# One landing buffer instead of two for the gathered token rows

## What is computed

```python
kv  = einsum('bhsd,bhse->bhde', k, v); out = einsum('bhsd,bhde->bhse', q, kv)
x   = (out / rms(out) * g_norm)  reshaped to (4608, 512)

logits = x @ w_gate + modality_bias[modality_id]        # 8 experts
e_idx  = argmax(logits);  gate_w = softmax(logits)[e_idx]
for e in range(8):                                      # each token goes to one expert
    h = maximum(x[e_idx == e] @ w1[e], 0)               # 512 -> 1024
    out[e_idx == e] = gate_w * (h @ w2[e])              # 1024 -> 512

out = (sigmoid(x @ w_gate2) * (x @ w_val)) @ w_out      # 512 -> 1536 -> 512
```

## Time and profile before

| | |
|---|---|
| median of 3 runs | 1508.95 us |
| the profiled execution's own time | 1508.95 us, of which its span 1507.2 us and 1.75 us around it |
| PE busy | 1386.6 us, 92% of the span |
| DVE busy | 906.8 us, 60% |
| ACT busy | 442.5 us, 29% |
| POOL busy | 303.1 us, 20% |
| granted clock, mean over the span | 0.956 |

### The profile page before, as it was taken

One profiled execution on the slowest core, in us unless ns is written; L12 is line 12 of the kernel. 1 busy time (PEld: TensorE's weight loads), 2 busy tenths in 40 slices (PEclk: granted clock), 3 DMA queues, 4 the chain that ended last, 5 costly groups with the idle time before them and its releaser, 6 DMA issues.

```text
span 1507.2 us, 25225 instructions
## 1 busy us (share of the span) xinstructions
PE 1386.6 (92%) x8270; PEld 1141.1 (76%) x8271; DVE 906.8 (60%) x1509; ACT 442.5 (29%) x766; POOL 303.1 (20%) x364
## 2 busy tenths in 40 slices
PE   4776379999999999979899999999999999999997
PEld 4565358878888888757678888888888888888885
DVE  3565776677758784456775557555575555655541
ACT  4555122222222222324432214211142112422221
POOL 0055324444444444212110001100011000110011
PEclk9777689999999999979999999999999999999999
DMA  9783256577747765459967443374426544144420
GB/s 329 290 311 126 88 163 183 169 211 212 204 147 223 208 197 146 121 128 354 336 233 202 147 151 121 128 201 147 147 78 168 173 158 155 42 175 147 147 77 28
DMA packets 132433, 262.68 MB, mean 174 GB/s; under 512 B 20200, under 2 KB 85736, under 8 KB 126208
## 3 DMA queue, kind: packets, MB, share of 16 engines
q1 hardware_dynamic: 71200, 199.41, 39.7%
q10 hardware_dynamic: 49952, 32.50, 8.3%
q0 software_dynamic: 11200, 29.69, 5.9%
HBM read 179.44 MB, written 51.73 MB: 153 GB/s over the span
## 4 chain that ended last, share of the span: by engine, by line
PE 80%; DVE 6%; DMA 5%; issue 4%; ACT 3%; SPq 1%; DVEq 1%; ACTq 0%; POOL 0%; POOLq 0%
PE ps L1547 30%; PE ps L1527 18%; PE ps L1497 13%; PE ps L1484 12%; DMA mixes<-mix 2%; PE ps L1406 2%; PE ps L1419 2%; PE ps L1517 1%; PE ps L1383 1%; DMA graw<-in_moe_w_val 1%; DMA vt<-in_v 1%; DMA raw<-in_moe_w 1%; DVE ew L957 1%; ACT qp L726 1%; DVE ew L963 0%
## 5 line engine op out<-in xcount | busy, mean ns | idle before, releaser
L1547 PE MATMUL ps<-a_hi,st 128*128 128x512 f32 x1344 | 421.5, 389 | 0.8 <-DVE u L1328 0.8
L1547 PEld LDWEIGHTS ps<-a_hi,st 128*128 128x128 f32 x1344 | 252.3, 188 | 54.0 <-DVE a_lo L1289 1.5
L1527 PE MATMUL ps<-wo,shi 128*128 128x512 f32 x864 | 268.5, 392 | 6.2 <-DVE slo L1298 5.4
L1547 PE MATMUL ps<-a_lo,st 128*128 128x512 f32 x672 | 261.4, 389 | 0.0
L1484 PE MATMUL ps<-ew,xhi 128*128 x640 | 200.3, 394 | 12.1 <-DVE xlo L1144 12.1
L1497 PE MATMUL ps<-ew,hhi 128*128 x640 | 200.8, 395 | 9.1 <-DVE hlo L1169 9.1
L1527 PEld LDWEIGHTS ps<-wo,shi 128*128 128x128 f32 x864 | 162.5, 189 | 44.4 <-issue 5.2
L671 POOL DMA_INDIRECT out<-ot,out_tok x36 | 35.9, 998 | 717.7 <-ACT ot L834 711.9
L1527 PE MATMUL ps<-wo,slo 128*128 128x512 f32 x432 | 170.0, 393 | 0.0
L1484 PEld LDWEIGHTS ps<-ew,xhi 128*128 128x128 f32 x640 | 122.0, 191 | 38.3 <-issue 12.9
L1497 PEld LDWEIGHTS ps<-ew,hhi 128*128 128x128 f32 x640 | 121.9, 191 | 35.9 <-issue 10.4
(11 more groups left out here) (221 smaller groups left out, 1811.8 us busy)
## 6 DMA issues: line engine op xcount, KB each, us to landing
st<-mixes SPq DMA_DIRECT2D x48, 1792.0 KB, 7.2
raw<-in_moe_w SPq DMA_DIRECT2D x64, 512.0 KB
hq<-h ACTq DMA_DIRECT2D x160, 128.0 KB
mixes<-mix SPq DMA_DIRECT2D x24, 512.0 KB, 8.7
xg<-xs ACTq DMA_DIRECT2D x158, 64.0 KB
kt<-in_k SPq DMA_DIRECT2D x8, 1152.0 KB, 9.2
vt<-in_v SPq DMA_DIRECT2D x8, 1152.0 KB, 12.6
qt<-in_q SPq DMA_DIRECT2D x8, 1152.0 KB, 9.0
```

The costliest lines, as they stand in the source:

```text
L1527: last = mm(ps[:, 4 + m, :], s[:, rows], wo[f // 2][:, w, f % 2], start=(f == 0 and w == 0 and s is shi[slot]), stop=(f == GC - 1 and s is ...
L1547: last = mm(bank_of(f, idx), st[f % 2][:, at:at + 128], x[:, idx, k, :], start=(k == 0 and w == 0 and x is a_hi), stop=(k == 1 and w == 1))
```

## The change

The two buffers `xs0` and `xs1` become one, `xs`, in the place of `xs0`, which `graw` does not touch. `gather_x(t)` now waits until the quarters of tile t-1 have landed (`x_in` of the other parity), from tile 1 on; its wait on `sorted_in` goes, since the quarters of t-1 can only have been issued after the gather of t-1 had landed. SP's wait on `xt_made` ahead of `load_glu(0)` goes too, since no gather buffer lies under `graw` any more.

```diff
-    xs1 = Place(ahead.at)("xs1", [128, D], F32)
     graw = ahead("graw", [128, 2, DC, 256], F32)
-    xs = [Place(ahead.at)("xs0", [128, D], F32), xs1]
+    xs = Place(ahead.at)("xs", [128, D], F32)
...
-                engine.dma_start(xg[32 * g:32 * g + 32], xs[t.p][:, 128 * g:128 * g + 128]).then_inc(x_in[t.p], 16)
+                engine.dma_start(xg[32 * g:32 * g + 32], xs[:, 128 * g:128 * g + 128]).then_inc(x_in[t.p], 16)
...
             tiles_used = sp.value_load(used[0:1, 0:1], min_val=FULL, max_val=NT)
-            sp.wait_ge(xt_made, tiles_used)
             load_glu(0)
...
             def gather_x(t):
-                if not isinstance(t.n, int) or t.n > 1:
-                    when(x_in[t.p], 64 * t.half)
                 if not isinstance(t.n, int) or t.n > 0:
-                    when(sorted_in, 32 * t.n)
+                    when(x_in[1 - t.p], 64 * (t.half + t.p))
...
-                        out=xs[t.p][:, HALF * n:HALF * n + HALF], out_offset=None, in_=x_rows,
+                        out=xs[:, HALF * n:HALF * n + HALF], out_offset=None, in_=x_rows,
```

## The result

The changed kernel takes 1569.0 us in the median of four runs (1564.3 to 1570.8), against 1509.2 (1505.5 to 1510.0) before: 1.040 times the time, 95% interval 1.037 to 1.043, or 60 us more. The forecast was 1516.5 with a range to 1529. The direction was right; the size was eight times too small, and what came is the rival "locked throughout", at twice the price that I had worked out for it.

A forecast was written before the change was run, and what follows sets the result against it. PE was taken as the bound, with a gather setting the end only at the expert stage's opening. Terms 3.4 - 0.5 + 4.5 + 0.5 = 7.9, rounded down to +7.5 on 1508.95, gave 1516.5 us; range 1510 to 1529.

The forecast's parts named there:

- locked throughout: Rival: the gather-quarters ring sets the pace in all three stretches with weight loads, 1537 us; chance 0.13 (throughout or nearly).
- What bounds the kernel: Whole kernel: PE holds 80% of the chain and is fully busy 335 to 560 us, so stalls reaching it add time.
- The opening: Start of the expert stage, tile 1: seat_x waits for tile 0's quarters, +3.4 us, less 0.5 from a quicker weight load.
- The ring in quiet stretches: Loop without weight loads: quarters, POOL's wake and next gather take 9.2 us, shorter than a 10.9 us step; costs nothing.
- The usual step with weights: Loop steps with weight loads: the late gather finds the weights through, so the new wait is covered to within 1 us.
- the example's gather: Loop, after the quarters issued at 352.13: second gather out at 359.0, landing at 361.7 or perhaps 363, next quarters at 363.13.
- Where the cover ends: From about 480 us, quarters meeting weights make a 12.3 us ring; six tiles at 1.4 us, less cover, about +4.5.
- The waits at PE: Between 480 and 560 us, PE was expected to wait on hlo or xlo some 4 to 5 us in sum.
- `graw` and POOL's fewer waits: Earlier graw load is already hidden, zero, at most +1 us; one semaphore wait less per gather on POOL, zero.
- a rival at 1532: Loop with weights: a late gather keeps its 5.2 us, ring 12.1 us in 23 tiles, about 1532; no separate chance given.

The follow-up runs named there:

- the first half refill: Changed kernel, but each half of the gather waits only for the two quarters that read its half of xs; 1518.8 us, ratio 1.007.

## Why the prediction was wrong, step by step

*What bounds the kernel* was right: PE, with no reserve between 335 and 560 us, so that a stall would be new time.

*The opening* was right in kind: +3.4 - 0.5 forecast, 4 us (1 to 7) measured with the wait on tile 1 alone, and 4.4 us from the first gather to the first `down` in the traces (37.3 against 32.9). One part I had missed. In the changed kernel the chain of the opening reads:

```profile
186.68 0.20 POOL seat_x L612
...
188.93 4.83 DMA xs<-x_rows,seat_x
...
195.74 2.21 DMA xg<-xs
...
204.61 4.59 DMA raw<-in_moe_w
```

The gather of tile 1 lands after 4.8 us instead of 2.8, and it now runs beside the store of the gate values (SP issued it at 188.79; 18 KB; its queue had 528 packets between 188 and 194 us). All seven kernels with the new wait and a whole refill, in which the second gather goes out 0.1 us behind this store, have 4.2 to 4.8 us; the one with the first half refill issues it 0.4 us ahead of the store (186.20 and 186.56), and it lands after 2.9. The weight load landed in 4.6 us instead of 5.5, 0.9 us gained where I had taken 0.5.

*The ring in quiet stretches* was costed at 9.2 us and is 10.4, since its gather lands after 3.8 us and not 2.7. That it costs nothing there held with 0.5 us to spare, and the wait on the last four tiles alone shows the zero. But I had counted on 1.6 us of recovery a step; with 0.5 the quarters do not get back to their old place ahead of the loads.

*The usual step with weights* is the step that failed. I wrote that there the new wait is covered to within 1 us, and let only six tiles lock. I had taken the quarters' landing at its quietest, 2.19 us from the opening, and the late gather's at 2.7, "with 2.7 us of its own". In the ring the gather runs beside the `hq` transfers of its step, 3.9 us, shown by the 2.8 with `hq` made small. With 3.9 the example's gather, issued at 359.0, lands at 362.9, next to the quarters at 363.13: hardly 0.2 us are left, and that only if the quarters are still at their quietest. They are not: issued on the gather's landing and no longer right behind `hq`, they meet the loads and take 4.1 to 6.6 us in 24 of 25 steps.

*Where the cover ends* had the mechanism right, quarters that meet the weights and are late again in the next step, but the price was 1.4 us a tile where the turn shown has 3.2 (14.1 less 10.9) and the 25 steps with loads 2.7 in the mean, and the extent was six tiles where it was all 25. In part the cause of the extent is in the same paragraph of the prediction: the lock keeps itself up. I said so, and then gave it a beginning at 480 us for which no row spoke; a state that keeps itself up has to be expected from the first step that reaches it. The rest is where the new wait puts the quarters: 0.5 us ahead of the loads instead of 2.2, so each of the last two groups began with a long step.

*The waits at PE* were taken as the whole cost. In the kernel whose PE waits again and again its busy time also rose by 13 us, 11.6 of them between 475 and 640 us, where the granted clock was 0.96 instead of 1.00. I had no term for this.

*`graw` and POOL's fewer waits* at zero were right.

*The rule of the Trainium skill* on turns between queues ("DMA: Bandwidth & Descriptors", "Queues, rings and completion order") led me to a rival at 1532, by a gather that stays at 5.2 us however late it is issued. That term did not come: most of the gathers in the ring land after 3.4 to 4.4 us. It was the quarters that stayed slow, with 1.1% of the engines beside a weight load's 70.6%. That is no contradiction of the rule, which promises turns and not equal shares: the section has an engine drain a whole packet, typically some 9 to 17 descriptors, from one queue before it switches. No row here shows where such a packet ends, so the traces do not test it.

*The chances*: 0.13 stood on the case that came, and even its price, 1537, was half of the loss. The range ended at 1529, inside the case it should have covered.

## What to carry to other kernels

When a double buffer is made single, write down the ring that this closes (every issue, wake and landing in it) and compare it with the step it must fit into, taking each landing from rows where the other transfers of that step are in flight, not from quiet ones; here 9.2 us on quiet rows was 14.1 in truth against a step of 10.9. Look, too, at where in the step the new wait puts each transfer, and what is issued just behind it there. If the ring is longer anywhere and its own delay brings on the collision that made it long, expect it in every step of that kind. Before paying for a second buffer, try refilling the one by halves with a semaphore each: it shortened the ring enough to cost nothing.

## What the runs showed that I had not expected

- A loss that only begins above the step is steep: by the ratios, half-size weights took back 50 of 60 us, small `hq` transfers 46, the first of the two half refills 50. Each took between 2 and 3 us out of a ring that had 3.2 too much.
- 64 KB transfers inside SBUF took 2.2 us to land when alone, up to 5.8 us when issued between the two 512 KB loads of a pair from DRAM; over the first 2.5 us they had 1.1% of the DMA engines, the load 70.6%.
- A gather issued 0.1 us behind a store of 18 KB in small packets landed after 4.2 to 4.8 us in seven kernels, and after 2.9 us when issued 0.4 us ahead of it; that these two are cause and effect rests on their times alone, and no run removed the store.
- Moving the weight split behind the transpose cost 40 us with two buffers, in a loop whose DVE is busy 78% (93.72 of 120 us, rows 2): the order of an engine's list weighed more than its load.
